# Where tile 1's convolution, the low weight parts and seven squares are computed, and which queue issues the first loads, in a fused convolution and two-layer kernel

## The reference

```python
w = softmax(weight_gen, axis=-1)                  # exp(w - max) / (sum + 1e-9), over 7 taps
x_pad = zeros of 6 rows ahead of x, per batch
out[b, s, head] = sum over k of w[b, s, head, k] * x_pad[b, s + k, head]   # 8 heads of 24 columns
x = out.reshape(8192, 192)
h = max(x @ w_in1, 0);  x = (h * h) @ w_out1      # first layer
h = x @ w_in2;          out = (h * cos(h)) @ w_out2   # second layer
```

## Time and profile before

| | before |
|---|---|
| median of three executions | 1219.65 us |
| the profiled execution | 1220.16 us |
| its span in the profile | 1218.4 us |
| TensorE busy, share of the span | 1177.9 us, 97% |
| VectorE | 977.7 us, 80% |
| ScalarE | 808.5 us, 66% |
| GpSimd | 365.6 us, 30% |
| chain that ended last, by engine | PE 86%, DVE 8%, ACT 3% |

### The profile page before, as it was taken

How to read it: one execution, slowest core, us unless ns; L and a number is a source line. 1 busy time by engine, 2 the same in 40 slices (tenths; PEclk the granted TensorE clock), 3 DMA queues, 4 the chain that set the end, 5 groups by cost and what they waited for, 6 DMA issues and landing times.

```text
span 1218.4 us, 25324 instructions
## 1 busy us (share of the span) xinstructions
PE 1177.9 (97%) x9725; PEld 1108.1 (91%) x9725; DVE 977.7 (80%) x1525; ACT 808.5 (66%) x1467; POOL 365.6 (30%) x247
## 2 busy tenths in 40 slices
PE   3889999999999999999999999999999999999997
PEld 2677889899999999999999999999999999999986
DVE  6887788887878778787877878787787878878786
ACT  3486776666767666676766667676676767676665
POOL 2946445115070421507042160704306070000000
PEclk9899999999999999999999999999999999999999
DMA  7332011111011111100111110011111000100000
GB/s 167 81 92 65 9 41 20 34 27 34 14 24 29 22 34 27 34 14 17 35 24 34 27 34 12 16 37 25 33 28 33 12 16 4 25 1 14 1 14 14
DMA packets 112983, 37.29 MB, mean 31 GB/s; under 512 B 101600, under 2 KB 110816, under 8 KB 112864
## 3 DMA queue, kind: packets, MB, share of 16 engines
q1 hardware_dynamic: 111520, 34.94, 13.9%
q10 hardware_dynamic: 1344, 0.74, 0.3%
HBM read 23.84 MB, written 6.29 MB: 25 GB/s over the span
## 4 chain that ended last, share of the span: by engine, by line
PE 86%; DVE 8%; ACT 3%; issue 1%; DMA 1%; SPq 0%; DVEq 0%; POOL 0%; ACTq 0%; POOLq 0%
PE y L526 45%; PE h L526 41%; DVE h L1136 1%; DVE h L1159 1%; DVE turns L1140 1%; ACT turns L928 1%; DVE g_lo L1177 1%; ACT g_hi L946 1%; DMA xc<-in_x_dram 1%; DVE x L1126 0%; ACT relu L901 0%; DVE g_lo L1173 0%; DVE stat L1028 0%; DVE stat L1021 0%; DVE wd_lo L1090 0%
## 5 line engine op out<-in xcount | busy, mean ns | idle before, releaser
L526 PE MATMUL y<-g_hi,wo 64*128 64x512 f32 x3030 | 698.6, 396 | 2.0 <-issue 1.5
L526 PE MATMUL y<-g_lo,wo 64*128 64x512 f32 x2020 | 525.4, 393 | 0.0
L526 PEld LDWEIGHTS y<-g_hi,wo 64*128 64x128 f32 x3030 | 423.3, 185 | 28.1 <-DVE xa_lo L1165 3.3
L450 POOL TENSOR_TENSOR tap<-xc,gen 128x768 f32<-128x768 f32 x105 | 163.4, 1562 | 568.5 <-DVE xd_lo L1148 562.5
L526 PEld LDWEIGHTS y<-g_lo,wo 64*128 64x128 f32 x2020 | 310.1, 185 | 6.5
L526 PE MATMUL h<-xa_hi,wa_hi 64*128 64x512 f32 x1016 | 277.1, 404 | 10.9 <-DVE g_lo L1173 7.3
L928 ACT ACTIVATE turns<-turns 128x512 f32<-128x512 f32 x239 | 151.3, 633 | 200.3 <-DVE turns L1140 199.3
L526 PE MATMUL h<-xa_hi,wa_lo 64*128 64x512 f32 x1016 | 269.3, 393 | 0.0
L526 PE MATMUL h<-xa_lo,wa_hi 64*128 64x512 f32 x1016 | 268.6, 392 | 0.0
L1159 DVE TENSOR_TENSOR h<-h,turns 128x512 f32<-128x512 f32 x239 | 166.6, 697 | 123.4 <-ACT turns L928 122.5
L1136 DVE SCALAR_TENSOR_TENSOR h<-h,relu 128x512 f32<-128x512 f32 x256 | 178.2, 696 | 68.0 <-ACT relu L901 65.5
(11 more groups left out here) (99 smaller groups left out, 1075.0 us busy)
## 6 DMA issues: line engine op xcount, KB each, us to landing
xc<-in_x_dram SPq DMA_DIRECT2D x60, 240.0 KB
out_dram<-arena SPq DMA_DIRECT2D x64, 64.0 KB, 1.9
xt_a<-x_blocks SPq DMA_DIRECT2D x224, 16.0 KB, 1.8
arena<-in_moe_w_out_dram SPq DMA_DIRECT2D x16, 192.0 KB, 3.4
arena<-in_moe_w_in_dram SPq DMA_DIRECT2D x16, 128.0 KB, 2.4
out_dram<-arena SPq DMA_DIRECT2D x60, 32.0 KB, 1.7
xt_d<-x_blocks SPq DMA_DIRECT2D x112, 16.0 KB, 1.8
arena<-in_moe_w_in_dram SPq DMA_DIRECT2D x16, 64.0 KB, 3.0
```

Of the source, the lines that this page charges most:

```text
L450: pool.tensor_tensor(tap[:, k % 2, :].rearrange("p (r g) -> p r g", g=GROUP), rows[k], wk, ALU.mult).then_inc(pool_step, 1)
L526: return pe.matmul(o, w[rows, :], x[rows, :], start=start, stop=stop)
```

## The change

VectorE loses its `piece_lo` (but for the first two operations of piece 0, now written out) and makes tile 1's convolution instead: `convolve_second` puts one step after each of slots 1 to 11, two after slots 1 and 2 (`CONV_SLOTS`). It also scales the weights of that tile (`softmax` operation 4). GpSimd makes all other low parts (pieces 2 to 7 at the start, 8 to 10 between its `shift`s, 11 before tile 2's convolution, 12 to 15 after it). ScalarE scales the raw weights of all layer 2 pieces, converts pieces from slots 2, 4, 5, 6, 8, 9, 11, 13, 15, 18, 20, 22 on, spread over three slots from slot 9, and in slots 2 to 8 makes the square into `h1` too (`ACT_SQUARES`). Tile 1 is turned in slot 13 and split in slot 14. The second rows of input are loaded after two more pieces. Of the eight first input loads SyncE issues four (it had six), ScalarE four (two).

```diff
@@ -81,11 +81,11 @@
-        return (SLOTS - 5, SLOTS - 10)[t] if t < PEEL else TURN
+        return (SLOTS - 3, SLOTS - 10)[t] if t < PEEL else TURN
...
-        return (SLOTS - 4, SLOTS - 5)[t] if t < PEEL else SPLIT
+        return (SLOTS - 2, SLOTS - 5)[t] if t < PEEL else SPLIT
@@ -236,32 +238,43 @@
         WARM_UP = 12
-        HI_AT = {4: 2, 5: 4, 6: 6, 7: 8, 8: 9, 9: 11, 10: 13, 11: 14, 12: 16, 13: 18, 14: 22, 15: 25}
+        LATE = 4
+        ACT_SQUARES = (2, 3, 4, 5, 6, 7, 8)
+        CONV_SLOTS = (1, 1, 2, 2, 3, 4, 5, 6, 7, 8, 9, 10, 11)
+        HI_AT = {4: 2, 5: 4, 6: 5, 7: 6, 8: 8, 9: 9, 10: 11, 11: 13, 12: 15, 13: 18, 14: 20, 15: 22}
         HI_AFTER = {}
...
             for op in range(3):
-                HI_AFTER.setdefault(n + op * (n > SLOTS), []).append((pc, op))
-        LO_AT = {2: 2, 4: 4, 5: 6, 6: 8, 7: 10, 8: 12, 9: 14, 10: 18}
-        POOL_LO = (3, 11, 12, 13, 14, 15)
-        LO_AFTER = {}
-        for pc, n in LO_AT.items():
-            LO_AFTER.setdefault(n, []).extend([(pc, 0), (pc, 1)])
-            LO_AFTER.setdefault(n + 1, []).append((pc, 2))
+                HI_AFTER.setdefault(n + op * (n > 8), []).append((pc, op))
+        CONV_AFTER = {}
+        for k in range(TAPS):
+            for op in range(2 if k else 1):
+                CONV_AFTER.setdefault(CONV_SLOTS[2 * k - 1 + op if k else 0], []).append((k, op))
...
         LOADS = [0, 2, 5, len(PARTS) - 1]
-        SOFTMAX_AFTER = {0: [(1, 2), (1, 3)]}
+        SOFTMAX_AFTER = {0: [(1, 2), (1, 3), (1, 4)]}
         SOFTMAX_AFTER.update({n: [(n - 1, 0)] for n in range(3, 10)})
...
+        def wait_squared(eng, n):
+            early = sum(k <= n for k in ACT_SQUARES)
+            if n in ACT_SQUARES:
+                eng.wait_ge(early_square, early)
+            else:
+                eng.wait_ge(square_ready, n + 1 - early)
         def gen_range(part):
@@ -323,14 +336,16 @@
-            for q in quarters:
+            for q, part in parts:
                 if q * JJ >= HALO:
                     rows(q, 0, BLOCK)
+                    continue
+                eng.wait_ge(halo_zeroed, 1)
+                if part == B:
+                    starts(q)
                 else:
-                    eng.wait_ge(halo_zeroed, 1)
-                    starts(q)
-                    for b in range(B):
-                        rows(q, b * BLOCK // B + 1, (b + 1) * BLOCK // B)
+                    rows(q, part * BLOCK // B + 1, (part + 1) * BLOCK // B)
@@ -394,7 +409,7 @@
             load_gen(sp, 0, (0, 1))
-            load_first_rows(sp, (0, 1))
+            load_first_rows(sp, ((0, 0), (0, 1), (0, B), (1, 0)))
             for pc in range(RING):
@@ -402,10 +417,10 @@
             load_gen(sp, 2)
-            for pc in range(RING + 2, PL + 2):
+            for pc in range(RING + 2, PL + 4):
                 load_piece(pc)
             load_rows(2)
-            for pc in range(PL + 2, PIECES):
+            for pc in range(PL + 4, PIECES):
                 load_piece(pc)
@@ -441,17 +456,18 @@
                     pool.wait_ge(x1_turned, 2 * t)
+                    pool.wait_ge(x1_ready, t - 1)
                 if counted(t - 1):
...
                     if k >= 2:
-                        pool.wait_ge(pool_step, STEP * (t - 1) + 2 * k - 1)
+                        pool.wait_ge(pool_step, STEP * (t - 2) + 2 * k - 1)
                     pool.tensor_tensor(tap[:, k % 2, :].rearrange("p (r g) -> p r g", g=GROUP), rows[k], wk,
...
                         continue
-                    pool.wait_ge(pool_step, STEP * (t - 1) + 2 * k)
+                    pool.wait_ge(pool_step, STEP * (t - 2) + 2 * k)
                     if k < TAPS - 1:
@@ -495,19 +511,22 @@
             piece_lo(1, 2)
-            for op in range(3):
-                piece_lo(3, op)
-            scale(1)
-            pool.wait_ge(gen_scaled, 2)
-            pool.wait_ge(x_loaded, FIRST_X + NEXT_X)
-            convolve(1)
+            for pc in range(2, PL):
+                for op in range(3):
+                    piece_lo(pc, op)
             for part in range(2, len(PARTS) - 1):
                 shift(part)
+                if part < 5:
+                    for op in range(3):
+                        piece_lo(PL + part - 2, op)
+            for pc in range(PL + 3, PL + LATE):
+                for op in range(3):
+                    piece_lo(pc, op)
             scale(2)
...
             convolve(2)
-            for pc in POOL_LO[1:]:
+            for pc in range(PL + LATE, PIECES):
                 for op in range(3):
@@ -880,7 +899,7 @@
                 last = act.activation(hi, w, ACT.Copy, scale=by)
-                if l and pc in POOL_LO:
+                if l:
                     last = act.activation(w, w, ACT.Copy, scale=by)
@@ -896,9 +915,12 @@
                     act.wait_ge(up1_done, n + 1)
-                    if counted(n - 1):
-                        act.wait_ge(square_ready, n - 1)
+                    if n >= 2:
+                        wait_squared(act, n - 2)
                     act.activation(relu[:, b, :], h1[b], ACT.Relu).then_inc(relu_done, 1)
+                    if n in ACT_SQUARES:
+                        act.wait_ge(relu_done, n + 1)
+                        act.activation(h1[b], relu[:, b, :], ACT.Square).then_inc(early_square, 1)
                 if live(m):
@@ -974,7 +996,7 @@
             load_gen(act, 0, (2, 3))
-            load_first_rows(act, (2, 3))
+            load_first_rows(act, ((2, 0), (3, 0), (1, 1), (1, B)))
             for part in range(2):
@@ -1020,6 +1042,8 @@
                                       op=ALU.add).then_inc(gen_sum[part], 1)
+                elif op == 4:
+                    scale(part)
                 else:
@@ -1071,32 +1095,32 @@
-            def piece_lo(pc, op):
...
+            def scale(part):
+                dve.wait_ge(inv_ready, part + 1)
+                dve.tensor_tensor(gen_view(part), gen_view(part), spread(part), ALU.mult).then_inc(gen_scaled, 1)
+            def convolve_second(k, op):
+                weights = gen[:, JJ * GEN:2 * JJ * GEN].rearrange("p (r k) -> p r k", k=TAPS)
+                total = x1[:, 0:JJ * DM]
+                done = 2 * k - 1 + op if k else 0
                 if op == 0:
-                    last = low(wa_lo[l][:, cols], stage_a[:, r, :], wa_hi[l][:, cols], by[0])
-                elif op == 1:
-                    last = low(wd_lo[rows, cols], stage_d[rows, r, :], wd_hi[rows, cols], by[0])
+                    if k == 0:
+                        dve.wait_ge(gen_scaled, 2)
+                        dve.wait_ge(x_loaded, FIRST_X + NEXT_X)
+                    if k >= 2:
+                        dve.wait_ge(second_step, done - (k > 2))
+                    dve.tensor_tensor(tap[:, k % 2, :].rearrange("p (r g) -> p r g", g=GROUP),
+                                      xc[:, k * DM:(k + JJ) * DM].rearrange("p (r g) -> p r g", g=GROUP),
+                                      weights[:, :, k:k + 1].to_broadcast([P, JJ * HEADS, GROUP]),
+                                      ALU.mult).then_inc(second_step, 1)
                 else:
-                    low(wo[l][:, fs, DM:2 * P], stage_o[:, r, :, DA:DM], wo[l][:, fs, DA:DM], by[1])
-                    last = low(wo[l][:, fs, 2 * P:2 * DM], stage_o[:, r, :, 0:DA], wo[l][:, fs, 0:DA], by[1])
-                last.then_inc(piece_ready[pc], 1)
+                    dve.wait_ge(second_step, done)
+                    if k == 1:
+                        dve.wait_ge(x1_turned, 2)
+                    dve.tensor_tensor(total, tap[:, 0, :] if k == 1 else total, tap[:, k % 2, :],
+                                      ALU.add).then_inc(x1_ready if k == TAPS - 1 else second_step, 1)
@@ -1131,7 +1155,7 @@
                 c = (i - C2) % 2
-                if live(n):
+                if live(n) and n not in ACT_SQUARES:
                     dve.wait_ge(relu_done, n + 1)
@@ -1183,12 +1207,16 @@
                 softmax(0, op)
-            dve.wait_ge(inv_ready, 1)
-            dve.tensor_tensor(gen_view(0), gen_view(0), spread(0), ALU.mult).then_inc(gen_scaled, 1)
+            scale(0)
             dve.wait_ge(gen_scaled, 1)
             convolve_first()
-            for op in range(2):
-                piece_lo(0, op)
+            dve.wait_ge(piece_hi[0], 1)
+            dve.tensor_tensor(wa_lo[0][:, 0:PIECE], stage_a[:, 0, :], wa_hi[0][:, 0:PIECE],
+                              ALU.subtract).then_inc(piece_ready[0], 1)
+            dve.wait_ge(piece_hi[0], 2)
+            dve.wait_ge(piece_ready[0], 1)
+            dve.tensor_tensor(wd_lo[0:DD, 0:PIECE], stage_d[0:DD, 0, :], wd_hi[0:DD, 0:PIECE],
+                              ALU.subtract).then_inc(piece_ready[0], 1)
             for part in range(2):
@@ -1198,8 +1226,8 @@
                 slot(n // SLOTS, n % SLOTS, n // SLOTS % 2)
-                for pc, op in LO_AFTER.get(n, ()):
-                    piece_lo(pc, op)
+                for k, op in CONV_AFTER.get(n, ()):
```

(29 more changed lines are left out.)

## The result

The changed kernel took 1209.24 us, median of four executions (1207.38 to 1209.68); the kernel before took 1219.89 us in the same series (1219.41 to 1220.80). The medians are 10.65 us apart, where 10.7 were forecast. The ratio of the means is 0.9909, 95% interval 0.9892 to 0.9926, which is 11.1 us less. The profiled execution took 1209.44 us, span 1207.6; against the span of before, 1218.4, that is 10.8.

The account below looks back on a forecast made before the run. From relu 2 to 17 TensorE was held by waits for late VectorE results and the low clock that followed. Terms 9.7 + 0 + 1.0 = 10.7 us off 1220.16 gave 1209.5, forecast median 1209 us, range 1203.5 to 1216.

Parts of the forecast that it names:

- the stretch: Relu of slot 2 to relu of slot 17: 12.6 us gone, 3.0 new, net 9.7 us taken; relu 17 at 76.9.
- Low clock: Relu 2 to 17: 10.7 us at 1.2 GHz cost TensorE some 5.3 us, which would go.
- Waits: TensorE, relu 2 to 17: waits of 1.99, 1.78, 1.65 and 1.86 us go, 7.3; new ones add 3.0.
- Low parts and convolution: Low parts to GpSimd end the 1.99 us wait; tile 1's 13 convolution steps on VectorE take 1.3 us each.
- Rival 2: Slots 1 to 3, 9 to 11: steps wait for GpSimd, 4.6 us more; 1213 to 1215; 0.19 together with rival 5.
- Squares: Slots 2 to 8, on ScalarE: each adds 0.48 us; chain 2.45 instead of 2.06 us, hidden under TensorE's 2.57.
- Slots 17 to 28: After the head: ScalarE's rounds set these slots, no change, 0 us, between -1 and +1.
- Tile 2's convolution: GpSimd ends near 99, transpose at slot 22 about 103.7: reserve falls to 4 to 5 us, nothing waits.
- Rival 5: Tile 2's convolution 5 us later than worked out, slot 22 waits: 1211 to 1213; 0.19 together with rival 2.
- First loads: Kernel start: inputs land sooner, TensorE's start follows one to one; 1.0 us gained, bounds 1.9 gained to 1.0 lost.
- Rival 1: Start: inputs land no sooner, transfer being the bound; 1210 to 1211; 0.57 together with the forecast.
- Rivals 3 and 4: 3: ScalarE and VectorE keep up everywhere, 1204 to 1206 (0.12); 4: TensorE stays at 1.2 GHz through head, about 1234 (0.12).

Follow-up runs that it names:

- the quarters: The kernel before with GpSimd's instructions for tile 1's convolution cut into four of a quarter each, same work: 1214.52 us, ratio 0.9961.
- after: The changed kernel as made, against the kernel before: 1209.24 us, ratio 0.9909.
- the conversions spread out: Changed kernel with 19 warm-up transposes, seven transposes in slot 18 and every weight piece's high-part conversions over three slots: 1204.26 us, ratio 0.9875.
- after with the old loads: The changed kernel with the first input loads dealt as before, SyncE issuing six and ScalarE two: 1208.05 us, ratio 0.9907.
- the short warm-up: Kernels with 12 warm-up transposes; the changed kernel with 19 instead took 1206.06 us, ratio 0.9891.
- both idle times filled: Changed kernel with 19 warm-up transposes, seven in slot 18, piece 8 spread: 1204.79 us; also with loads dealt as before: 1205.32; or every piece spread: 1204.26.
- the filling: Seven identity transposes at the head of slot 18; added alone to the changed kernel: 1207.11 us, ratio 0.9901.

## Why the prediction was right, and where it was not

**What bounds the kernel, and the stretch: right.** Net 9.7 us were forecast, 9.42 measured, relu 17 at 76.9 without the loads or near 76 with them: 76.12. The mechanism was tested by itself, with the quarters. By busy and idle time two of its terms were mis-sized and cancel:
- Low clock: 5.3 us forecast, as half of 10.7; the busy time fell by 3.96. The low stretches before, by their windows:

```profile
38.62:42.03 3.41, 3.41 (x18) 2.80 (x15) 1.71 (x4) 0.00 (x0) 3.25 (x3) 0.50 0.20 55
48.86:52.27 3.41, 3.29 (x14) 2.86 (x16) 3.38 (x6) 0.70 (x2) 3.28 (x2) 0.50 0.07 19
59.10:62.51 3.41, 3.41 (x17) 2.87 (x17) 3.27 (x7) 1.21 (x3) 1.44 (x2) 0.50 0.71 196
```

  They make 10.23 us, and TensorE was busy for 10.11 of them, so the level cost at most half of that, 5.1 us, if no matmul takes more than twice as long there: close to the forecast. Why the busy time fell by less is in part the way it is counted: successive matmuls' records overlap (0.39 us long, 0.23 apart), so the end of the matmul ahead of each wait counts as busy, and after has more waits, though short ones. The rest is not shown.
- Waits: 7.3 gone and some 3.2 new make 4.1; idle time fell by 5.46. The four new waits named by slot are 1.56 us where 0.8 at slot 5, 0.9 at slot 11 and 0.7 at slot 12 were forecast: 0.25, 0.56 and 0.45 (and 0.30 at slot 4). The wait of 1.18 moved to slot 16 and stayed, as forecast. ScalarE was as late as worked out (4.02 us at slot 8, forecast 1.65 + 2.33), but less of it reached TensorE, which runs up to two slots ahead. The waits that the forecast put at slots 13 and 15 did not come.

**Low parts and convolution: right.** The 13 steps, from 30.45 to 62.21 us, took 0.95 to 1.44 us, two products recorded together 2.25; mean 16.13 / 13 = 1.24 against 1.3. Rival 2, contention that eats the convolution, is out: leaving 11 steps away shortened the stretch by 0.35 us. Not foreseen was that GpSimd pays too (1.50 for 0.73); its pieces were early enough for that.

**Squares: cost right, place wrong, use not asked.** A square adds 0.54 us against 0.48. But the chain from relu to the end of `g_lo` was forecast at 2.45 us, "hidden while TensorE's slot is 2.57"; it is 2.57 (slot 2: 32.02 to 34.59), and no cover is left. TensorE's slot n + 2 waits for `g_lo` of slot n, so the chain is the likeliest reason why slots 3 to 8 take 2.7 to 3.0 us: they do so without the convolution too (2.82 a slot) and with the conversions spread out. No run tested the chain by itself. The prediction took the squares' use as given; they shorten the stretch by 0.7 us.

**Slots 17 to 28: forecast 0 within 1, just outside.** The stretch from relu 17 to 28 is 1.3 us shorter (52.13 for 53.45). This is given back by relu 32, where the two kernels are as far apart as at 17 (10.72 and 10.65). Up to relu 20 0.18 us are lost: relu 18 to 19 takes 1.03 us longer, with the level low for longer than before (mean granted clock 0.77 for 0.89), relu 19 to 20 1.01 less. Where the level did not fall, after with the old loads, relu 17 to 20 took 12.56 us, 2.3 less than before.

**Tile 2's convolution: right.** Reserve 5.2 us, forecast 4 to 5; transpose at 103.0, forecast 103.7; no wait. Rival 5 is out.

**First loads: this step failed, though the number looked right.** Forecast 1.0 us as TensorE's start follows the landing "one to one". In the profiled pair relu 2 does come 1.23 us sooner, but with the old dealing it came 1.03 sooner too (32.22 for 33.25), and the kernel before's first product was a late one. The edit by itself gained 0 in the kernel before; undone in after it cost 0.25 us at relu 17 in the trace, and nothing that the times could show. The landing is 1.0 us sooner on average, as forecast; the wrong part is "one to one". Between landing and end stood the low level of the first slots and the wait for `wd_lo`, and in the kernels with the short warm-up relu 2 came at 31.55 to 32.95 with the new dealing and at 32.22 to 33.82 with the old; the ranges overlap. With both out of the way the term is 0.5 us by the medians, 0.7 by the traces. The Trainium skill, "DMA: Bandwidth & Descriptors", section "Issuing engines are not separate DMA queues", says that more issuers save issue time alone. The trace agrees: the landing's 1.0 us is under the issue time saved, which is 1.53 us (up to 1.85 was forecast), as the last input row was issued by 5.56 and now by 4.03 on ScalarE's queue:

```profile
3.34 0.69 ACTq L336 DMA_DIRECT2D xc<-in_x_dram  x1
```

Rival 1 thus came near in what the term is worth, but not by its mechanism: the inputs did land sooner.

**The total: in part luck.** It came out to 0.1 us with that term worth next to nothing. The other edits gave somewhat more than their 9.7: 11.2 us with the old dealing (1208.05 for 1219.28), 9.9 with the new (1209.24 for 1219.16, of another series). In the profiled pair the lead is 1.23 us at relu 2 and 9.42 in the stretch, and nothing is added behind relu 17. The lead at relu 2 comes from when the low level of the first slots ended (matmuls take about 0.4 us again from 31.85 before and from 30.38 after). Behind relu 17 up to 2.5 us more were there, in slots 18 and 19, in the traces without a fall of the level (relu 17 to 20 in 12.55 to 13.30 us for 15.05). Such a fall would explain most of the 2.3 us by which the executions of after differ: its profiled execution, with the fall, took 1209.44 us, that of after with the old loads, without it, 1207.13. The other executions left no trace, so this stays argued.

**Rivals 3 and 4.** Small waits remain, so ScalarE and VectorE don't keep up everywhere, but 1.56 us in all put the truth nearer to rival 3 than the forecast stood. The level stayed at 2.4 GHz in slots 3 to 16, as forecast. Past the start it fell at one place only, slot 18, behind a wait that stood there before as well and behind which it fell before too (0.89).

## What to carry to other kernels

When a vector instruction's duration grows beside another engine, look at which instruction of that engine it ends with: shortening those instructions is a test of the cause by itself, and here nearly half of the whole gain (4.8 of 10.65). Look for idle time just ahead of the first matmuls: filling 1.65 us brought relu 17 forward by 2.97. Work moved to another engine can lengthen the chain that the next slots wait for: price the chain and not only the engine's load. An earlier landing is a gain only if no later wait and no fallen clock stands between it and the end: undo that one edit before its term is believed.

## What was not expected of the hardware

- The wait between VectorE and GpSimd goes both ways, and the first to start keeps its time: 0.95 and 1.50 us at 43.2, 1.22 and 0.73 at 34.2 to 34.5.
- The page's clock column can read 1.00 where the matmuls run at the low level. After's window from 22 to 30 us shows 1.00, while its matmuls there take 0.6 to 0.79 us, as those of the kernel before from 25.3 to 31.7 do, where the column says 0.50 (windows, after and then before, columns as in rows 1). In such a stretch the durations decide.

```profile
22.00:30.00 8.00, 7.90 (x22) 5.09 (x23) 5.12 (x10) 2.89 (x5) 7.28 (x13) 1.00 0.67 178
```

```profile
25.30:31.70 6.40, 6.40 (x20) 4.33 (x19) 3.61 (x7) 2.46 (x4) 6.04 (x10) 0.50 0.60 165
```

- Behind much the same wait at slot 18 (1.36 to 1.54 us) the level fell in eight of the nine kernels profiled without the filling, for a shorter or a longer time, and in one it did not. After spreads over 2.3 us in four executions; of the three versions with both idle times filled two spread over 0.6, the third over 1.6.
